# Three units of the second perceptron moved into the last block of the first

## The reference

```python
def _moe_ref(x, w_in, w_out):          # first perceptron
    h = x @ w_in
    g = where(h >= 1, h, where(h <= -1, 0.0, (h + 1) ** 2 / 4))
    return g @ w_out

def _moe2_ref(x, w_in, w_out, a, b):   # second perceptron
    h = x @ w_in
    P = a[0] + a[1] * h + a[2] * h**2 + a[3] * h**3
    Q = 1.0 + abs(b[0]) * abs(h) + abs(b[1]) * h**2
    g = P / (Q + 1e-06)
    return g @ w_out
```

## Time and profile before

| | |
|---|---|
| median of 3 runs | 979.9 us (979.46 to 980.42) |
| profiled execution | 982.7 us |
| its span, first to last instruction | 981.0 us |
| PE busy | 925.1 us (94%) |
| DVE busy | 746.5 us (76%) |
| ACT busy | 570.6 us (58%) |
| POOL busy | 255.0 us (26%) |
| mean granted PE clock | 0.976 of full speed |

### The profile page before, as it was taken

One profiled execution on the slowest core, in us unless ns is written; L12 is line 12 of the kernel. 1 busy time (PEld: TensorE's weight loads), 2 busy tenths in 40 slices (PEclk: granted clock), 3 DMA queues, 4 the chain that ended last, 5 costly groups with the idle time before them and its releaser, 6 DMA issues.

```text
span 981.0 us, 12883 instructions
## 1 busy us (share of the span) xinstructions
PE 925.1 (94%) x4626; PEld 751.1 (77%) x4626; DVE 746.5 (76%) x909; ACT 570.6 (58%) x725; POOL 255.0 (26%) x138
## 2 busy tenths in 40 slices
PE   4589899999999999999999969999999999999996
PEld 3467678888888888888887748888888888888884
DVE  8567777777667667767556689888888888888883
ACT  5344444443444444344344488788788787887872
POOL 3233330000000000100025434325335234243223
PEclk9699889999999999999999999999999999999999
DMA  5423322211211221121033230001010010010000
GB/s 144 129 74 113 96 63 69 65 33 33 82 33 48 67 64 33 33 81 42 1 88 88 82 96 1 1 33 32 0 64 0 0 64 0 21 43 0 32 1 35
DMA packets 27510, 48.68 MB, mean 50 GB/s; under 512 B 5312, under 2 KB 8384, under 8 KB 27456
## 3 DMA queue, kind: packets, MB, share of 16 engines
q1 hardware_dynamic: 27456, 48.00, 16.5%
HBM read 36.18 MB, written 9.44 MB: 47 GB/s over the span
## 4 chain that ended last, share of the span: by engine, by line
PE 78%; DVE 11%; ACT 4%; issue 4%; SPq 1%; POOL 1%; DMA 0%; POOLq 0%; ACTq 0%; DVEq 0%
PE acc L1096 19%; PE acc L1052 16%; PE h_pair L1036 16%; PE at_pair L1074 9%; PE h_pair L1074 9%; DVE t L837 3%; PE at_pair L979 2%; PE at_pair L997 2%; DVE growth L768 2%; PE at_pair L992 2%; PE at_bank L1006 1%; DVE g L844 1%; ACT t L592 1%; ACT w_hi L586 1%; SPq L334 1%
## 5 line engine op out<-in xcount | busy, mean ns | idle before, releaser
L490 POOL TENSOR_TENSOR g_lo<-g,g_hi 128x1024 fp32r<-128x1024 f32 x48 | 116.9, 2435 | 234.0 <-DVE t L872 229.5
L599 ACT CAST g_hi<-g 128x512 fp32r<-128x512 f32 x96 | 59.6, 621 | 187.6 <-DVE g L844 187.6
L837 DVE SCALAR_TENSOR_TENSOR t<-t 128x512 f32<-128x512 f32 x96 | 89.4, 931 | 89.8 <-ACT t L592 89.4
L592 ACT ACTIVATE t<-h_pair,half 128x512 f32<-128x512 f32 x96 | 65.8, 686 | 98.7 <-PE h_pair L1036 98.4
L1036 PE MATMUL h_pair<-x_hi,w_hi 128*128 128x512 f32 x288 | 115.4, 401 | 4.5 <-DVE g L844 2.5
L1052 PE MATMUL acc<-g_hi,w_hi 128*128 128x512 f32 x288 | 119.5, 415 | 0.0
L1052 PE MATMUL acc<-g_lo,w_hi 128*128 128x512 f32 x288 | 115.4, 401 | 0.0
L1096 PE MATMUL acc<-g_hi,w_hi 128*128 128x512 f32 x288 | 113.9, 396 | 1.5 <-POOL g_lo L490 1.4
L1052 PE MATMUL acc<-g_hi,w_lo 128*128 128x512 f32 x288 | 115.2, 400 | 0.0
L1036 PE MATMUL h_pair<-x_lo,w_hi 128*128 128x512 f32 x288 | 114.1, 396 | 0.0
L1036 PE MATMUL h_pair<-x_hi,w_lo 128*128 128x512 f32 x288 | 113.9, 395 | 0.0
(11 more groups left out here) (133 smaller groups left out, 2014.6 us busy)
## 6 DMA issues: line engine op xcount, KB each, us to landing
w_raw<-w SPq DMA_DIRECT2D x32, 384.0 KB, 3.4
f_in<-fC SPq DMA_DIRECT2D x48, 96.0 KB, 2.8
k_in<-kC SPq DMA_DIRECT2D x48, 96.0 KB, 2.4
q_in<-qC SPq DMA_DIRECT2D x48, 96.0 KB, 2.3
v_in<-vC SPq DMA_DIRECT2D x24, 192.0 KB, 2.6
mlp_out<-o_sb SPq DMA_DIRECT2D x18, 256.0 KB, 3.1
x_raw<-mlp_out SPq DMA_DIRECT2D x6, 768.0 KB, 4.4
outT<-o_sb SPq DMA_DIRECT2D x18, 256.0 KB, 2.0
```

Source lines behind the costliest of these rows:

```text
L490: nc.gpsimd.tensor_tensor(g2_lo[r][:, :, :], g2[r][:, :, :], g2_hi[r][:, :, :].bitcast(F32), ALU.subtract).then_inc(lo2_ready, 1)
L592: nc.scalar.activation(t1[n % 2][:, :], h1[n % 2], ACT.Relu, scale=0.5, bias=half[:, :]).then_inc(relu1_ready, 1)
L599: nc.scalar.copy(g1_hi[n % R1][:, :], g1[n % 2][:, :]).then_inc(hi1_ready, 1)
L837: nc.vector.scalar_tensor_tensor(out=t1[n % 2][:, :], in0=t1[n % 2][:, :], scalar=1.0, in1=t1[n % 2][:, :], op0=ALU.min, op1=ALU.mult).the ...
```

## The change

Units 0, 1 and 2 of the second perceptron (`EARLY = 3`) are taken out of the changeover and spread over the last block of the first one, from its steps 6, 9 and 12 on. All three put their h into `at_pair`, so unit 1 waits for the numerator of unit 0, and unit 2 for that of unit 1. The pieces of such a unit stand at these places, with t the step at which PE forms its h: in step t+1 ACT squares and takes the absolute value, and DVE forms the denominator; in step t+2 come ACT's line and guess and DVE's numerator; in step t+3 DVE's inverse and quotient; in step t+4 ACT's rounding and POOL's low part. The split of x for the second perceptron moves one step forward, to steps 3 to 5. The buffers are laid out so that the first three units have their own room beside the ring, but for the low part of unit 2, which waits for the last maximum of the first perceptron. Unit 3 follows in `h_pair` after the tile loop.

```diff
+EARLY = 3
+EARLY_FIRST = [6, 9, 12]
+X_FIRST = 3
...
+        def h2_of(n, m):
+            return at_pair if isinstance(n, int) and n < EARLY else h2[m % 2]
...
         def _(pool):
...
-                if SPLIT_X <= t < SPLIT_X + KT:
-                    split_x2(0, t - SPLIT_X)
-            for k in range(STEPS2.index(TILES - 1) + 1, PIECES):
-                split_w2(k)
-            run2(pool, rational_step, 1 + UNITS, UNITS + 2, peel=1)
+                if X_FIRST <= t < X_FIRST + KT:
+                    split_x2(0, t - X_FIRST)
+                if t - 4 in EARLY_FIRST:
+                    rational_lo(EARLY_FIRST.index(t - 4), EARLY_FIRST.index(t - 4))
+            split_w2(PIECES - 3)
+            rational_lo(EARLY - 1, EARLY - 1)
+            split_w2(PIECES - 2)
+            split_w2(PIECES - 1)
+            run2(pool, rational_step, 1 + UNITS, UNITS + 2, done=EARLY, peel=1)
...
         def _(act):
...
                 if stage == 0:
                     copy_keys(i)
-                if n < N1:
-                    spline_hi(n)
+                if t - 2 in EARLY_FIRST:
+                    rational_line(EARLY_FIRST.index(t - 2), EARLY_FIRST.index(t - 2))
+                spline_hi(n)
...
+                if t - 1 in EARLY_FIRST:
+                    rational_in(EARLY_FIRST.index(t - 1), EARLY_FIRST.index(t - 1))
+                if t - 2 in EARLY_FIRST:
+                    rational_guess(EARLY_FIRST.index(t - 2), EARLY_FIRST.index(t - 2))
+                if t - 4 in EARLY_FIRST:
+                    rational_hi(EARLY_FIRST.index(t - 4), EARLY_FIRST.index(t - 4))
+                if t in STEPS2:
                     split_w2(STEPS2.index(t))
-            act.wait_ge(coef_loaded, 32)
-            act.wait_ge(b_abs_set, 1)
-            rational_step(0, 0, [PIECES - 3])
-            rational_step(0, 1, [PIECES - 2])
-            copy_acc1(BLOCKS - 1)
-            rational_step(0, 2, [PIECES - 1])
+            rational_hi(EARLY - 1, EARLY - 1)
+            rational_step(0, EARLY, [PIECES - 3, PIECES - 2])
+            rational_step(0, EARLY + 1, [PIECES - 1])
...
         def _(dve):
...
                 spline_lo(n)
+                t = n - (N1 - TILES)
+                if t - 1 in EARLY_FIRST:
+                    denominator(EARLY_FIRST.index(t - 1), EARLY_FIRST.index(t - 1))
+                if t - 2 in EARLY_FIRST:
+                    numerator(EARLY_FIRST.index(t - 2), EARLY_FIRST.index(t - 2))
+                if t - 3 in EARLY_FIRST:
+                    inverse(EARLY_FIRST.index(t - 3), EARLY_FIRST.index(t - 3))
+                    quotient(EARLY_FIRST.index(t - 3), EARLY_FIRST.index(t - 3))
...
         def rational_first(n, m, blk):
...
-                if late(n, 2):
+                if late(n, EARLY + 1):
                     pe.wait_ge(h2_read, n - 1)
-                elif n == 1:
+                elif n == EARLY:
                     pe.wait_ge(g1_ready, N1)
+                elif n > 0:
+                    pe.wait_ge(h2_read, n)
...
                 if n >= LAG1:
                     spline_second(n - LAG1)
+                if n - (N1 - TILES) in EARLY_FIRST:
+                    m = EARLY_FIRST.index(n - (N1 - TILES))
+                    rational_first(m, m, 0)
...
-            rational_step(0, 0)
             spline_second(N1 - 2)
-            rational_step(0, 1)
+            rational_step(0, EARLY)
             spline_second(N1 - 1)
-            for off in range(2, LAG2 + 2):
+            for off in range(EARLY + 1, LAG2 + 2):
                 rational_step(0, off)
```

More of the change, by code:

```diff
@@ L151, in build @@
         s2 = [lay.tile(f"s2_{r}", [P, UW, NB]) for r in range(2)]
[L152 to L155, removed]
+        g2 = [lay.tile(f"g2_{r}", [P, UW, NB]) for r in range(EARLY)]
+        g2_hi, g2_lo = [], []
+        for r in range(EARLY):
             g2_hi.append(lay.tile(f"g2_hi{r}", [P, UW, NB], F32R))
+            assert lay.at <= ring_at
             g2_lo.append(lay.tile(f"g2_lo{r}", [P, UW, NB], F32R))
-            own += lay.at <= ring_at
+        g2.append(lay.tile(f"g2_{EARLY}", [P, UW, NB]))
+        g2_hi.append(lay.tile(f"g2_hi{EARLY}", [P, UW, NB], F32R))
+        g2_lo.append(lay.tile(f"g2_lo{EARLY}", [P, UW, NB], F32R))
         assert lay.at <= nc.sbuf_usable_end - 128
@@ L484, in rational_lo @@
                     pool.wait_ge(multiplied2, n - R2 + 1)
-                elif r >= own:
+                elif n == EARLY - 1:
+                    pool.wait_ge(g1_ready, N1)
+                elif n >= EARLY:
                     pool.wait_ge(multiplied1, N1)
-                if have2(n + 2):
+                if late(n, EARLY) and have2(n + 2):
                     pool.wait_ge(inv_done, n + 2)
@@ L667, in rational_step @@
                     rational_in(n, m)
-                if have2(n - 2):
+                if late(n - 2, EARLY) and have2(n - 2):
                     rational_hi(n - 2, (off - 2) % R2)
+                if isinstance(n, int) and n == EARLY:
+                    copy_acc1(BLOCKS - 1)
                 if ends_block:
@@ L851, in spline_lo, with denominator, inverse @@
                                         ALU.subtract).then_inc(lo1_ready, 1)
+            def denominator(n, m):
+                dve.wait_ge(sq_ready, n + 1)
+                dve.wait_ge(abs_ready, n + 1)
+                nc.vector.scalar_tensor_tensor(out=s2[m % 2][:, :, :], in0=s2[m % 2][:, :, :], scalar=b_abs[:, 1:2],
+                                               in1=g2[m % R2][:, :, :], op0=ALU.mult, op1=ALU.add).then_inc(den_ready, 1)
+            def inverse(n, m):
+                s, t = s2[m % 2][:, :, :], t2[m % 2][:, :, :]
+                dve.wait_ge(guess2_ready, n + 1)
+                nc.vector.scalar_tensor_tensor(out=s, in0=s, scalar=1.0 + EPS, in1=t, op0=ALU.add, op1=ALU.mult).then_inc(e_done, 1)
+                dve.wait_ge(e_done, n + 1)
+                nc.vector.scalar_tensor_tensor(out=t, in0=s, scalar=2.0, in1=t, op0=ALU.subtract, op1=ALU.mult).then_inc(inv_done, 1)
@@ new lines, in numerator @@
+            def numerator(n, m):
+                h = h2_of(n, m)[:, :].rearrange("p (c t) -> p c t", c=UW)
+                g = g2[m % R2][:, :, :]
+                dve.wait_ge(lin_ready, n + 1)
+                nc.vector.tensor_tensor(g, h, g, ALU.mult).then_inc(x1_done, 1)
+                dve.wait_ge(x1_done, n + 1)
+                nc.vector.scalar_tensor_tensor(out=g, in0=g, scalar=a_bc[:, 1:2], in1=h,
+                                               op0=ALU.add, op1=ALU.mult).then_inc(h2_read, 1)
@@ L853, in rational_step, with quotient @@
+            def quotient(n, m):
+                g = g2[m % R2][:, :, :]
+                dve.wait_ge(inv_done, n + 1)
+                dve.wait_ge(h2_read, n + 1)
+                nc.vector.scalar_tensor_tensor(out=g, in0=g, scalar=a_bc[:, 0:1], in1=t2[m % 2][:, :, :],
+                                               op0=ALU.add, op1=ALU.mult).then_inc(g2_ready, 1)
             def rational_step(base, off):
                 n, m, m1 = base * UNITS + off, off % UNITS, (off - 1) % UNITS
-                h = h2[m % 2][:, :].rearrange("p (c t) -> p c t", c=UW)
@@ L856, in rational_step @@
-                g, g_before = g2[m % R2][:, :, :], g2[m1 % R2][:, :, :]
-                s, s_before = s2[m % 2][:, :, :], s2[m1 % 2][:, :, :]
-                t_before = t2[m1 % 2][:, :, :]
+                earlier = late(n - 1, EARLY) and have2(n - 1)
                 if have2(n):
[L861 to L864, removed]
@@ L890, in _ @@
+                if earlier:
+                    inverse(n - 1, m1)
+                if have2(n):
+                    numerator(n, m)
+                if earlier:
+                    quotient(n - 1, m1)
             scan(0)
```

53 lines of the change are left out of this document (19 added, 34 removed).

## The result

| | before | changed |
|---|---|---|
| median | 980.16 us (979.46 to 980.48, 4 runs) | 990.61 us (990.45 to 992.02, 4 runs) |
| span of the profiled execution | 981.0 us | 990.3 us |
| mean granted PE clock | 0.976 | 0.973 |

The changed kernel is slower: the ratio is 1.0111, with a 95% interval of 1.0093 to 1.0128. The forecast was 988 us, that is 8.0 more; measured are 10.5 by the medians (the interval of the ratio gives 9.1 to 12.5) and 9.3 by the spans of the two profiled executions.

The account below looks back on a forecast made before the run. PE bounds most of the kernel, ACT and DVE the last block. Waits 20.1, restarts 0.9 and clock 1.6 make 22.6 us of new loss against 14.6 old: 8.0 slower, 988 us, range 976 to 995 (8 in 10).

Parts of the forecast that it names:

- the old bubble: PE's loss around the changeover in the kernel before: 14.6 us, of which 8.9 in waits and 3.5 in slow matmuls.
- The walk: Step-by-step timing of PE, ACT, DVE and POOL from unit 0 on: new loss 22.6 us against 14.6, 8.0 slower.
- nine places: PE waits at units 0, 1, 2, 3, 5, 6, 8, tile 94's second half and the first second half: 20.1 us.
- the first second half: First second half of a unit after the block: waits 0.6 us on ACT's copy of sums, starts about 598.6.
- Unit 0: At its start PE waits 2.5 us for POOL's third low part of x; ACT and DVE run dry over 5 us.
- Meetings: DVE instructions with two SBUF inputs held up by POOL instructions reading SBUF, in the last block: 6.1 us in all.
- rival 2: No change: in the last block the new DVE instructions miss POOL's; +1.9 us or less, 981; chance 0.10.
- one slow stretch, 1.6: Clock term: slow PE matmuls counted once, behind the 6.1 us wait before unit 2, costing 1.6 us.
- tile 94: Before its second half, PE arrives at 578.4 and waits until 581.3 for its low part, 2.9 us.
- Rival 3: Slower still: 1.9 us of slow matmuls behind each of five PE waits above 2.4 us; +15.9, 996; chance 0.10.
- three steps of the ring: ACT and DVE's repeating chain per tile in the last block, 4.58 us against PE's 4.16; three take 13.8 us.
- Rival 1: Faster: DVE's numerators keep ahead, units 1 and 2 start without waiting; 12.0 us faster, 968; chance 0.15.

Follow-up runs that it names:

- experiment 5: Changed kernel, on PE alone the first half of unit 0 put behind the first half of tile 87 instead of before it: 983.80 us, ratio 1.0047.
- experiment 3: Changed kernel, POOL's low part of a weight piece in the last block waits until DVE has squared the next tile: 985.02 us, ratio 1.0035.
- experiment 6: Changed kernel, POOL's weight pieces held until DVE's next square, first halves of units 0 to 2 each behind the next tile's first half: 977.86 us.
- the gate: Added wait: POOL's weight piece in the last block starts after DVE's square of the next tile; alone in the kernel before, 977.28 us.
- the places mended: Changed kernel's first halves of units 0, 1 and 2 on PE each moved behind the next tile's first half; with the gate, 977.86 us.
- experiment 1: Changed kernel, POOL's low part of the second perceptron's weights replaced by a memset to zero that reads no SBUF: 977.64 us, ratio 0.9967.
- experiment 2: Kernel before, POOL's low part of the second perceptron's weights replaced by the same memset to zero: 974.82 us, ratio 0.9937.
- Experiment 8: Changed kernel, 10, 11, 18 and 8 unused matmuls added on PE where it waits before units 0, 1, 2 and 3: 988.91 us, ratio 1.0092.
- experiment 7: Changed kernel, first halves of units 0, 1 and 2 on PE each behind the next tile's first half, POOL not held: 984.80 us, ratio 1.0043.

## Why the prediction was right, and where its sizes were off

*Direction and mechanism.* The early units do take the old bubble away, and PE waits more in the last block than it waited in the bubble. The walk put waits at nine places, and seven of them are there (not before the first second half and unit 5). The two causes it named for them, ACT and DVE run dry behind unit 0 and DVE behind POOL, were each taken away alone (experiments 5 and 3: 6.8 and 5.6 us) and together (6: 12.8). Of that the gate gives 3.3 to the kernel before as well, so the fair comparison is with that kernel and its gate: the loss is 10.5 us as it was, 7.7 with the gate in both, and 0.6 with the places mended too (977.86 against 977.28), which is none within the intervals. The two causes work on one another, so they cannot be given fixed shares: without the reads of the weight pieces the same places cost only 2.8.

*Unit 0.* 2.5 us walked for x, 2.6 measured. What it does is not the 2.6 us on PE but the 7.2 us that ACT idles, since tile 87's h stands behind it (experiment 5).

*Meetings.* They came where the walk had them, and at the lengths that it took from the nearest rows: 2.75 against 2.76 for the inverse, 1.37 against 0.69 + 0.75 for the low part. I had their price at 6.1 us in all (rival 2: +1.9 without them). With the weight pieces' reads gone the two kernels still differ by 2.8, so the price is some 7.6 by that; with the gate in both kernels, which leaves some meetings, 2.8 of the loss go. Experiments 1 and 2 shorten POOL's work as well, which leaves the figure uncertain by about as much as it is off.

*The clock was mis-sized.* The term "one slow stretch, 1.6" should have read four, 7.6 with their restarts. Waits of 2.35 to 2.6 us were enough this time; before, the shorter of the two with a slow stretch behind it was 2.9. At the same time the waits came out 3.5 us shorter than walked (16.6 against 20.1), mostly at unit 2 and tile 94: slow units 0 and 1 delay PE, which then waits less. Before unit 2 PE stands at 558.7 instead of the 555.6 walked, and the numerator is done at 563.2 instead of 561.65. So 5.4 us too little for the clock stand against 3.5 too much for the waits, and it is in part luck that the sum is off by no more than 2. Experiment 8 shows how the two hang together: with 5.7 us of slow matmuls less, the waits are 3.4 longer and the time 1.7 shorter. The first second half of a unit, forecast at 598.6, starts at 600.4. Rival 3 (+15.9, every slow stretch on top of the waits) had the stretches right and their price wrong.

*The rest.* Two sums of the working are slightly off and enter nothing else: the six instructions of a unit on ACT add up to 6.8 us, not 6.6, and three steps of the ring to 13.7, not 13.8. By the profiled executions the loss is 9.3 us, 1.3 over the sum, and by the medians 10.5; the difference between these two stays unexplained, it is that of single executions. *Rival 1* failed at the point it named: the starts of units 0, 1, 2 and 3 on PE are 21.0, 22.8 and 25.2 us apart, waits included, where some 20.6 was the most that still gained. With places and gate mended (experiment 6) it holds in part: 977.9, though not the 968 it stood for.

## What to carry to other kernels

Work put ahead of the data of a slower engine pair starves them: before moving a block of matmuls into a stage with slack on PE, look which engines set the pace there, and place it behind what feeds them, not before. The waits of PE in such a stage, and the slow clock behind them, add up to what is lost but do not tell what made it: with one taken away, another can grow. Follow the ring of the slower engines. And where GpSimd subtracts from SBUF beside a tight DVE chain, one more wait that holds it until DVE reads PSUM can be worth as much as the reordering with all its mending: the gate alone in the kernel before gives 977.3 us, the early units with gate and later places 977.9.

## What the runs showed of the hardware

- In the changed kernel a DVE instruction with two SBUF inputs that begins under a GpSimd subtraction ends about the same time behind it in every row looked at: 0.55 us for 512 columns (square of 533.50), 1.08 for 1024 (inverse of 545.88). The other way round, GpSimd waits as well: its weight piece takes 2.31 us when it begins beside a denominator (532.96) and 2.75 beside the first half of the inverse (544.80) instead of 1.84.
- A memset on GpSimd of the same 768 columns does not meet DVE at all (experiment 1).
- Slow matmuls do not follow from the length of a wait alone. Behind gaps of 2.6, 2.8, 4.5 and 2.6 us the changed kernel has them four times; in the kernel of experiment 5, unit 3 behind a gap of 2.6 us takes 4.21 us, without a slow stretch. In the kernel of experiment 7 a gap of 2.1 us was followed by slow ones: of the nine matmuls of the tile that begins at 551.94, the last five stand 0.43 us apart.
